# Rotary attention before two gated layers on one core: the order of the lone attention's casts, row sums and first weights

## The reference

```python
q_rot, k_rot = (rotate(q), rotate(k))          # x1*cos - x2*sin | x1*sin + x2*cos, B 2, H 8, S 576, D 64
scores = scale * np.matmul(q_rot, k_rot.transpose(0, 1, 3, 2))
scores = scores - np.max(scores, axis=-1, keepdims=True)
attn = np.exp(scores)
attn = attn / (np.sum(attn, axis=-1, keepdims=True) + 1e-09)
out = np.matmul(attn, v)                       # then tokens x 512
h = x @ w_in;  x = (h * (1.0 / (1.0 + np.exp(-h)))) @ w_out       # first layer, d_ff 2048
h = x @ w_in;  x = np.where(h > 0.0, h, np.exp(np.minimum(h, 0.0)) - 1.0) @ w_out   # second
```

## Time and profile before

| | us |
|---|---|
| median of 3 runs (lowest, highest) | 583.26 (582.5, 583.9) |
| the profiled execution | 582.42 |
| its span, first to last instruction | 580.6 |
| PE busy | 541.5 |
| DVE busy | 295.8 |
| ACT busy | 349.8 |
| POOL busy | 346.2 |

### The profile page before, as it was taken

The page is one execution under the profiler, slowest core; times in us unless marked ns, Lnnn a source line. Parts: engine busy times, 40 slices in busy tenths (PEclk is TensorE's granted clock), DMA queues, the critical chain, the costliest instruction groups (busy, mean ns, idle before and its releaser), DMA issues.

```text
span 580.6 us, 9268 instructions
## 1 busy us (share of the span) xinstructions
PE 541.5 (93%) x3308; PEld 529.8 (91%) x3308; DVE 295.8 (51%) x505; ACT 349.8 (60%) x726; POOL 346.2 (60%) x284
## 2 busy tenths in 40 slices
PE   1586789999999999999999999999999999999998
PEld 1576779999999999999999999999999999999997
DVE  4669965663336775325664425776434550047500
ACT  2677858875457676555875546766555773356531
POOL 3877778957763654754664564445444666656662
PEclk9989999999999999999999999999999999999999
DMA  6576662635544425434434433323433544434450
GB/s 239 185 190 174 158 197 73 174 112 193 156 114 137 137 90 164 146 102 144 129 109 140 112 108 111 109 76 114 143 103 98 145 128 128 128 109 128 124 157 28
DMA packets 43229, 77.16 MB, mean 133 GB/s; under 512 B 5296, under 2 KB 12848, under 8 KB 43184
## 3 DMA queue, kind: packets, MB, share of 16 engines
q1 hardware_dynamic: 41456, 74.21, 43.6%
q10 hardware_dynamic: 1728, 2.36, 1.1%
HBM read 63.57 MB, written 2.36 MB: 114 GB/s over the span
## 4 chain that ended last, share of the span: by engine, by line
PE 74%; DVE 14%; ACT 5%; issue 3%; DMA 2%; POOL 1%; SPq 0%; ACTq 0%; DVEq 0%; POOLq 0%
PE banks L895 60%; PE banks L860 4%; PE banks L832 4%; PE banks L818 3%; PE banks L820 2%; DVE neg_max L612 2%; DVE banks L686 2%; DVE act_buf L684 2%; ACT act_buf L487 1%; DVE pt_lo L619 1%; ACT prob L435 1%; DMA k_st<-k_raw 1%; PE banks L839 1%; DMA k_raw<-k 1%; DVE g_lo L619 1%
## 5 line engine op out<-in xcount | busy, mean ns | idle before, releaser
L321 POOL TENSOR_TENSOR w_lo<-w_raw,w_hi 128x512 fp32r<-128x512 f32 x192 | 247.0, 1288 | 204.3 <-ACT w_hi L475 203.6
L475 ACT CAST w_hi<-w_raw 128x512 fp32r<-128x512 f32 x189 | 117.1, 621 | 40.3 <-PE banks L895 36.2
L895 PE MATMUL banks<-x_lo,w_hi 128*128 128x384 f32 x384 | 130.5, 340 | 1.0 <-DVE g_lo L692 0.7
L895 PE MATMUL banks<-g_lo,w_hi 128*128 128x384 f32 x384 | 129.0, 336 | 0.0
L895 PE MATMUL banks<-x_hi,w_lo 128*128 128x384 f32 x384 | 128.6, 335 | 0.0
L895 PE MATMUL banks<-g_hi,w_lo 128*128 128x384 f32 x384 | 128.5, 335 | 0.0
L895 PE MATMUL banks<-x_hi,w_hi 128*128 128x384 f32 x384 | 128.5, 335 | 0.0
L895 PE MATMUL banks<-g_hi,w_hi 128*128 128x384 f32 x384 | 128.4, 334 | 0.0
L619 DVE TENSOR_TENSOR pt_lo<-banks,pt_hi 128x512 fp32r<-128x512 f32 x60 | 41.3, 689 | 94.7 <-ACT pt_hi L443 94.3
L818 PE MATMUL banks<-k_st,q_one 128*128 128x288 f32 x160 | 53.3, 348 | 30.9 <-DVE q_two L666 14.2
L435 ACT ACTIVATE prob<-banks,neg_max 128x576 f32<-128x576 f32 x72 | 53.5, 743 | 45.9 <-DVE neg_max L612 45.6
(11 more groups left out here) (74 smaller groups left out, 722.6 us busy)
## 6 DMA issues: line engine op xcount, KB each, us to landing
w_raw<-w SPq DMA_DIRECT2D x192, 256.0 KB, 2.7
q_raw<-q SPq DMA_DIRECT2D x11, 384.0 KB, 3.2
q_one<-q_raw SPq DMA_DIRECT2D x44, 96.0 KB, 2.6
k_raw<-k SPq DMA_DIRECT2D x7, 576.0 KB, 4.2
k_st<-k_raw SPq DMA_DIRECT2D x28, 144.0 KB, 2.5
v_raw<-v SPq DMA_DIRECT2D x8, 320.0 KB, 3.0
out<-act_buf ACTq DMA_DIRECT2D x12, 192.0 KB, 2.6
q_two<-q_raw SPq DMA_DIRECT2D x22, 96.0 KB, 2.3
```

Source lines behind the costliest of these rows:

```text
L321: nc.gpsimd.tensor_tensor(w_st[LO][:, slot, :], w_raw[:, slot, :], w_st[HI][:, slot, :].bitcast(F32), ALU.subtract).then_inc(w_lo_done, 1)
L475: nc.scalar.copy(w_st[HI][:, slot, :], w_raw[:, slot, :]).then_inc(w_hi_done, 1)
L895: last = nc.tensor.matmul(dst, w_st[wp][:, slot, m * P:(m + 1) * P], src[xp][:, tile, :], start=start and n == 0, stop=stop and n == 2)
```

## The change

It has five parts. (1) ACT's `queries_hi` and `keys_hi` of pairs 2 to 4 move: queries from the odd head's first tile (n = 3, 9, 15) to the even head's last (n = 8, 14, 20), keys from n = 5, 11, 17 to n = 9, 15, 21. POOL's `values_lo` moves behind the rotations. (2) Epsilon lies in memory beside every row sum, and a `tensor_reduce` over the two takes the place of the `tensor_scalar`. (3) POOL, not DVE, makes the high parts of the first three weight units, and the rotation of pair 5's queries follows the low parts of those weights. (4) The low part of the first queries waits for one copy of ACT instead of two; PE and SP get the wait for the second. (5) At the end of the lone attention PE does five input-tile steps of units 0 to 2 ahead of the last value products, and DVE adds the outputs before it inverts the sums.

```diff
-        row_sum = sb("row_sum", [P, 2, QN, 2])
+        row_sum = sb("row_sum", [P, 2, QN, 2, 2])
@@ SP load_queries
+                if r == 2:
+                    sp.wait_ge(first_q_hi, 4)
@@ POOL
+            def first_weight_hi(n):
+                pool.wait_ge(w_in[n], 16)
+                nc.gpsimd.tensor_copy(w_st[HI][:, n, :], w_raw[:, n, :]).then_inc(first_w_hi, 1)
@@
+            values_lo(0)
             for p in range(3):
-                values_lo(p)
                 rope_queries(p + 2)
                 rope_keys(p + 2)
+                values_lo(p + 1)
                 queries_lo(p + 2)
+                if p:
+                    first_weight_hi(p - 1)
                 keys_lo(p + 2)
-            values_lo(3)
-            rope_queries(5)
+            first_weight_hi(2)
             for n in range(AHEAD):
                 weight_lo(n)
+            rope_queries(5)
             rope_keys(5)
@@ ACT, the loop of the lone attention (even head above, odd head below)
                     if t == 2 and p:
                         widen_sums(p - 1)
-                else:
-                    if t == 0 and p < 3:
-                        queries_hi(p + 2)
+                        queries_hi(p + 1)
+                else:
+                    if t == 0 and p:
+                        keys_hi(p + 1)
                     if t == 2 and p:
                         output_hi(p - 1)
-                    if t == 2 and p < 3:
-                        keys_hi(p + 2)
@@ DVE
-                nc.vector.tensor_scalar(sum_eps[:, :, :], row_sum[:, p % 2, :, :], EPS, None, ALU.add) \
+                if p == 0:
+                    dve.wait_ge(eps_set, 1)
+                nc.vector.tensor_reduce(sum_eps[:, :, :], row_sum[:, p % 2, :, :, :], AXES.X, ALU.add) \
@@
-                dve.wait_ge(first_q_hi, 2 * par + 2)
+                dve.wait_ge(first_q_hi, 2 * par + 1)
@@
-                if n in (11, 13, 15):
-                    first_weight_hi((n - 11) // 2)
@@
+            add_outputs(H - 2)
             invert_sums(H // 2 - 1)
-            add_outputs(H - 2)
@@ PE
                     pe.wait_ge(first_k_lo, i + 1)
+                    pe.wait_ge(first_q_hi, 2 * i + 2)
@@
-                hidden_unit(start, range(1))
                 if c == 0:
-                    hidden_unit(start, range(1, KT - 1))
+                    hidden_unit(start, range(2))
+                    hidden_unit(start + 1, range(2))
+                    hidden_unit(start + 2, range(1))
                     value_products(ahead - 1)
-                    hidden_unit(start + 1, range(KT - 1))
+                    hidden_unit(start + 2, range(1, 2))
+                    hidden_unit(start, range(2, 3))
                     spread_sums(ahead // 2 - 1)
-                    hidden_unit(start + 2, range(KT - 1))
+                    hidden_unit(start + 1, range(2, 3))
+                    hidden_unit(start + 2, range(2, 3))
```

More of the change, by code:

```diff
@@ L147, in build @@
         ident_zero, ident_ready = sem("ident_zero"), sem("ident_ready")
-        q_zero, pads_zero = sem("q_zero"), sem("pads_zero")
+        q_zero, eps_set, pads_zero = sem("q_zero"), sem("eps_set"), sem("pads_zero")
         k_scaled, q_scaled = sem("k_scaled"), sem("q_scaled")
@@ L435, in exp_tile @@
                 nc.scalar.activation(halves(prob[:, n % 3, :]), scores(n), ACT.Exp, bias=neg_max[:, n % 2:n % 2 + 1],
-                                     accum_out=row_sum[:, i // 2 % 2, t, i % 2:i % 2 + 1]).then_inc(exp_done, 1)
+                                     accum_out=row_sum[:, i // 2 % 2, t, i % 2, 0:1]).then_inc(exp_done, 1)
             def probs_hi(n):
@@ L664, in first_queries_lo @@
                 rows = rows_of[par]
-                dve.wait_ge(first_q_hi, 2 * par + 2)
+                dve.wait_ge(first_q_hi, 2 * par + 1)
                 nc.vector.tensor_tensor(q_two[par][rows, 0:CT], q_raw[0][rows, 0, :],
                                         q_one[par][rows, 0:CT].bitcast(F32), ALU.subtract).then_inc(first_q_lo, 1)
-            def first_weight_hi(n):
-                dve.wait_ge(w_in[n], 16)
-                nc.vector.tensor_copy(w_st[HI][:, n, :], w_raw[:, n, :]).then_inc(first_w_hi, 1)
             def hidden_mul(n):
@@ L714, in _ @@
                 nc.vector.memset(q_two[par][other_rows_of[par], :].bitcast(F32), 0.0).then_inc(q_zero, 1)
+            nc.vector.memset(row_sum[:, :, :, :, 1:2], EPS).then_inc(eps_set, 1)
             dve.wait_ge(sin_in, 16)
@@ L946, in _ @@
                 start, ahead = UNITS * c, H * (c + 1)
-                hidden_unit(start, range(1))
                 if c == 0:
-                    hidden_unit(start, range(1, KT - 1))
+                    hidden_unit(start, range(2))
+                    hidden_unit(start + 1, range(2))
+                    hidden_unit(start + 2, range(1))
                     value_products(ahead - 1)
-                    hidden_unit(start + 1, range(KT - 1))
+                    hidden_unit(start + 2, range(1, 2))
+                    hidden_unit(start, range(2, 3))
                     spread_sums(ahead // 2 - 1)
-                    hidden_unit(start + 2, range(KT - 1))
+                    hidden_unit(start + 1, range(2, 3))
+                    hidden_unit(start + 2, range(2, 3))
                 else:
+                    hidden_unit(start, range(1))
                     spread_sums(ahead // 2 - 1)
```

## The result

The changed kernel takes 597.27 us (median of 4 runs, 596.81 to 597.5), the kernel before 583.58 us beside it: a ratio of 1.0237 (95% interval 1.0214 to 1.0261), slower by 13.7 us. The forecast was 594.3 us, 11.0 us slower, with a range up to 598.0. Its direction, its place and its mechanism were right. One term, the price of the clock, was half of what came; the other errors are of some tenths of a microsecond.

The account below looks back on a forecast made before the run. Before 95 us DVE (47.6 to 78 us) and chains of waits bound it, afterwards PE. Periods and placements +9.0, tail -0.5, clock +2.7 gave +11.2 us: 593.6 on the profiled execution, 594.3 against the median; range 589.0 to 598.0.

Parts of the forecast that it names:

- the price of the clock: PE's granted clock falls to half in each of three new idle stretches, 0.9 us each, +2.7 us in all.
- The bound: From 95 us to the end PE is busy, so a delay to the layers' begin comes out nearly one to one.
- The way from key cast to score: From ACT's moved key cast over POOL, copy issue and landing to PE's scores: 5.5 us; tile 12 +3.75 us.
- Forward by 0.3 us through part (4): At score 0, DVE waits for one ACT copy only; everything up to the first placements comes 0.3 us earlier.
- The periods: Tile 12 to 18 and 18 to 24 take 17.3 us each, not 15.72 and 13.67; tile 24 is +9.0 us.
- The rival of a full clock: At the new waits the clock does not fall, idle stretches being somewhat shorter: 591.8 us; chance 0.17.
- The tail, gain 0.5 us: From tile 24 to the end of units 0 to 2, `spread_sums` starts earlier: 0.5 us gained.
- POOL's casts: Three weight casts moved to POOL take 1.0 us each, covered by the wait for the key cast up to 1.8 us.
- The sum: DVE's reduce does not wait beside POOL's work, winning 0.8 us; if it waited, the total is 0.8 us higher.
- late landings: At the three placements, copies land later than 5.5 us, 0.6 to 2.9 us more each: 596 to 603; chance 0.10.
- DVE's relief decides: From pair 2's key cast to score 12 the copies are in time, so the kernel gets faster: 579.5 us; chance 0.05.
- Only the first placement is late: Only tile 12 is late, as a freer DVE brings later casts earlier relative to PE: 583.6 us; chance 0.04.

Follow-up runs that it names:

- the filler: The changed kernel with 48 transposes of the identity, read by nobody, ahead of the scores of tiles 12, 18 and 24: 591.93 us, ratio 1.0128.
- the casts between the two places: Part (1) undone, first four weight loads behind pair 1's placements, plus query casts at n = 5, 11, 17, key casts at 6, 12, 18: 579.77 us.

## Why the prediction was right

*The bound.* Right: the 14.1 us lost by the end of the first units stood at the end, as 14.4.

*The way from key cast to score, 5.5 us.* Measured 5.3 three times; the issue taken at 0.64 us was 0.51. Tile 12 was forecast at 49.05 and came at 49.29, since the cast came 0.4 us later than the sum has it (43.98 for 43.55).

*Forward by 0.3 us through part (4).* Not seen here, and not settled. The idle 0.33 us is gone, and tile 6's copies were issued 0.8 us earlier (23.94 against 24.73). But they took 7.42 us, as SP's queue and the chain show, and landed 0.3 us later: score 6 at 31.49 against 31.22.

```profile
19.30 1.86 SPq L232 DMA_DIRECT2D w_raw<-w  x4
```
```profile
23.94 7.42 DMA k_st<-k_raw
```

With the weight loads moved behind them the same copies land in 2.5 us, so it is those loads that make the landing late. How late varies from execution to execution: in the four kernels with part (4) and the loads ahead, score 6 starts at 30.02, 30.53, 31.29 and 31.49 us, in the four without it at 30.92, 31.22, 31.55 and 31.86. A term of 0.3 us can't be read from one pair of these.

*The periods.* Forecast at 17.3 us with the full clock; with the clock held up by the filler they are 17.38 and 17.33. The relief of DVE's casts and sums was in front of a wait, as said; with part (1) undone, the periods of 13.8 and 13.3 us (forecast 13.2) show it.

*The clock, 0.9 us each.* The term that was mis-sized: 2.0, 1.4 and 1.9 us, together 5.3 where 2.7 was taken. Two of the three are above the upper bound of 1.65 that I gave. That bound came from one stretch of 3.3 us at half speed; after the waits here PE worked at 1.2 GHz for 5.6 us (49.3 to 54.9), 3.2 us (68.7 to 71.9) and 5.0 us (87.4 to 92.4). Each price stays below half of its stretch. Taking one stretch's length as a limit was the mistake. The mechanism, and that it comes in each wait, was right. The argument for it hung on one case, though: "at most 2.9 us after silence" came from the same single stretch, while in the first new wait the clock fell only 4.6 us after PE fell silent. The rival of a full clock is refuted as a description, while its 591.8 us is just what the filler kernel gives. The signs that hang on this term were off too: the third slice at 0.5 came at 86 us, not near 82, and the layers began at 93.5 us, not near 89.

*The tail, gain 0.5 us.* With part (1) undone it is 13.78 against 13.94 us, with the filler 13.36: between 0.2 and 0.6. As said, PE idles there for the last input tile, 0.73 us.

*POOL's casts.* 0.61 us each, below the 1.0 taken and at the estimate from the Trainium skill (GPSIMD Engine Reference, "3.1 Elementwise — side-by-side cycle accounting"). Hidden, as forecast. It is not 0.61 everywhere: with part (1) undone two of the three took 0.95 us, both overlapping a subtraction of DVE on two tiles in the SBUF (`x_lo`, from 49.30 and 63.06 us); no run tells whether that is the cause.

*The sum.* The reduce never stretched, 0.15 to 0.17 us in all twelve, which agrees with the Trainium skill (SBUF — State Buffer, "Who interferes with whom").

By terms, with the clock as measured, the sum is +9.0 - 0.5 + 5.3 = 13.8; with the 0.2 us by which tile 12 was later and 0.1 in the periods it is the 14.1 us found at the end of the first units. Measured over all are 14.4 on the profiled executions and 13.7 on the medians. Of the 3 us between forecast and median the clock is nearly all. That the range still held 597.27 is in part luck: its upper end was set by late landings, which did not come, not by a larger price of the clock. (The terms as printed give 594.4, not 594.3.)

*The rivals.* "DVE's relief decides" would need the way from cast to landing under 1.4 us; it was 5.3. Its number, 579.5, is near what comes once the late casts are taken back (580.9). "Only the first placement is late" is refuted by the two others. Late landings of more than 5.5 us did not come in the changed kernel, but copies that took 6.7 and 7.3 us did in kernels with the weight loads moved.

## What to carry to other kernels

A step moved later on an idle-looking engine must be priced by the whole way behind it: here 0.7 us of cast carried POOL's part, two DMA issues and a landing, 5.3 us, and the in-order queue of PE stood for all of it. Compare that way with the time until the consumer's turn in its own program order, not until its data are used on average. A stall that is seen on one engine (ACT waiting for POOL) is worth removing only if no other wait ends later; and bulk loads issued just ahead of small copies set when those land. Moving these loads carried the wait from tile 6 to tile 12 and on to tile 18, and spreading them ended it, yet the times of these versions are not told apart: a wait gone from the trace is not yet time gained.

## What was not expected of the hardware

- The granted clock fell as little as 2.3 us and as much as 4.6 us after PE fell silent, in one and the same execution (the changed kernel: silent from 62.8 and from 43.4 us, half speed from 65.1 and 48.0). In another kernel the fall came only as the silence ended: with the casts between the two places PE was silent from 24.2 to 26.53 us, and the clock was at 0.50 from 27 us, with PE already at work.
- How long PE's work stays at 1.2 GHz after silence varied between 3.2 and 5.6 us in that execution.
- SBUF to SBUF copies of 144 KB took 2.5 to 2.7 us to land in the median of each kernel, and 6.1 to 7.5 us with a megabyte of loads from HBM issued 4.6 to 4.8 us ahead of them. Where the megabyte was issued 8.8 us ahead, it was 3.4 us.
